# Gram products of two heads at once from a cleared buffer, in a one-core delta-rule attention and mixture kernel

## The reference, cut to what matters

```
B, H, S, D = 4, 8, 768, 48
k_n = k / (norm(k) + 1e-6)
for t in range(S):                       # state is [B, H, D, D], zero at first
    y[t]  = q[t] @ state
    state = state + beta[t] * outer(k_n[t], v[t] - k_n[t] @ state)
x = y as [3072, 384]
logits = x @ phi; d = softmax over tokens; c = softmax over the 32 slots
slots  = d.T @ x; slot_out = relu(slots @ w1[e]) @ w2[e];  x = c @ slot_out
h = x @ w_in; g = h * sigmoid(1.702 h); out = g @ w_out
```

## Time and profile before

| | |
|---|---|
| median of 3 runs | 500.15 us |
| profiled execution | 499.79 us, span 498.1 us |
| PE (matmul) busy | 462.5 us, 93% |
| PEld (weight load) busy | 344.1 us, 69% |
| VectorE (DVE) busy | 347.3 us, 70% |
| ScalarE (ACT) busy | 312.5 us, 63% |
| DMA moved | 59.20 MB, mean 119 GB/s |

### The profile page before, as it was taken

How to read it: one execution, slowest core, us unless ns; L and a number is a source line. 1 busy time by engine, 2 the same in 40 slices (tenths; PEclk the granted TensorE clock), 3 DMA queues, 4 the chain that set the end, 5 groups by cost and what they waited for, 6 DMA issues and landing times.

```text
span 498.1 us, 17806 instructions
## 1 busy us (share of the span) xinstructions
PE 462.5 (93%) x7422; PEld 344.1 (69%) x7422; DVE 347.3 (70%) x1126; ACT 312.5 (63%) x704; POOL 8.7 (2%) x21
## 2 busy tenths in 40 slices
PE   7889898978798899998999999999999999999997
PEld 4666675665566576665344788888788888887885
DVE  4985779999989998545652887566565656665662
ACT  3235657988869898875361776655656556556553
POOL 3000000000000000000000000000000000000000
PEclk8556888999989999999999999999999999999999
DMA  6911223666644434699999000100100100101001
GB/s 231 378 55 42 94 92 120 210 186 189 187 120 129 144 103 131 201 276 329 347 409 384 11 2 0 65 0 1 63 0 3 60 0 21 42 0 38 27 1 63
DMA packets 29800, 59.20 MB, mean 119 GB/s; under 512 B 3488, under 2 KB 12704, under 8 KB 29344
## 3 DMA queue, kind: packets, MB, share of 16 engines
q1 hardware_dynamic: 29728, 58.16, 34.4%
HBM read 53.43 MB, written 4.72 MB: 117 GB/s over the span
## 4 chain that ended last, share of the span: by engine, by line
PE 68%; DVE 17%; ACT 5%; issue 4%; DVEq 0%; ACTq 0%
PE bank L922 13%; PE bank L923 13%; PE bank L929 12%; DVE tmp L1273 5%; DVE tt L1278 5%; PE bank L889 4%; PE bank L612 3%; PE bank L552 3%; PE bank L625 2%; PE bank L819 2%; PE bank L794 2%; PE bank L541 2%; ACT zb L936 2%; ACT state L936 2%; DVE rr L1174 2%
## 5 line engine op out<-in xcount | busy, mean ns | idle before, releaser
L922 PE MATMUL bank<-g_h,wo_h 128*128 128x512 f32 x288 | 112.9, 392 | 0.1
L923 PE MATMUL bank<-g_h,wo_l 128*128 128x512 f32 x288 | 112.1, 389 | 0.0
L1497 DVE TENSOR_TENSOR g_l<-g,g_h 128x512 fp32r<-128x512 f32 x96 | 66.5, 693 | 64.6 <-ACT g_h L936 64.6
L936 ACT ACTIVATE g_h<-g 128x512 fp32r<-128x512 f32 x96 | 60.8, 634 | 69.2 <-DVE g L1492 69.2
L929 PE MATMUL bank<-g_l,wo_h 128*128 128x512 f32 x270 | 75.9, 389 | 0.0
L1492 DVE TENSOR_TENSOR g<-bank,sig 128x512 f32<-128x512 f32 x96 | 66.3, 691 | 13.1 <-ACT sig L1114 7.5
L936 ACT ACTIVATE zb<-bank 32x192 f32<-32x192 f32 x192 | 61.8, 322 | 17.2 <-PE bank L612 15.3
L1114 ACT ACTIVATE sig<-bank 128x512 f32<-128x512 f32 x96 | 57.2, 596 | 16.6 <-PE bank L889 16.2
L922 PEld LDWEIGHTS bank<-g_h,wo_h 128*128 128x128 f32 x288 | 54.1, 188 | 14.2 <-ACT res L936 2.6
L923 PEld LDWEIGHTS bank<-g_h,wo_l 128*128 128x128 f32 x288 | 54.1, 188 | 10.8
L1278 DVE TENSOR_TENSOR tt<-tt,tmp 128x126 f32<-128x126 f32 (+34 forms) x290 | 60.2, 250 | 0.0
(11 more groups left out here) (158 smaller groups left out, 485.7 us busy)
## 6 DMA issues: line engine op xcount, KB each, us to landing
slice<-in_w SPq DMA_DIRECT2D x48, 256.0 KB, 3.1
slice<-in_w SPq DMA_DIRECT2D x28, 384.0 KB, 7.0
kq<-in_kq_t SPq DMA_DIRECT2D x12, 512.0 KB, 6.6
kq<-in_kq_t SPq DMA_DIRECT2D x24, 256.0 KB, 3.1
vn<-in_v_nat SPq DMA_DIRECT2D x24, 192.0 KB, 3.1
out_t<-res SPq DMA_DIRECT2D x18, 256.0 KB, 2.1
kn<-in_k_nat SPq DMA_DIRECT2D x23, 192.0 KB, 2.7
win<-in_w_in SPq DMA_DIRECT2D x3, 1024.0 KB, 15.6
```

Source lines behind the costliest of these rows:

```text
L922: eng.matmul(acc[d][:], wo_h[:, f, cols], g_h[:, f % GR], start=(f == 0), stop=False)
L923: eng.matmul(acc[d][:], wo_l[:, f, cols], g_h[:, f % GR], start=False, stop=False)
L936: return eng.activation(out, src, ACT.Copy)
L1497: eng.tensor_tensor(g_l[:, f % GR], g[:, f % GR], g_h[:, f % GR].bitcast(F32), ALU.subtract).then_inc(s_gl, 1)
```

## The change

`kq` is split. k of 12 chunks and q of 4 chunks share a ring `kqa` of 16 places; a second buffer `sg` holds two chunks, [128, 2, 2 (a), 2 (k, q), 16 pairs, 32]. In its block a = 0 only partitions 0 to 63 are ever loaded and 64 to 127 stay zero (GpSimd clears them once); in block a = 1 the other way round. So one product with all 128 rows of k stationary and the 128 columns (two heads, k and q) of `sg` moving gives both heads' Gram products: 16 products of 128 columns in place of 32 of 64. This holds for chunks 4 to 23; chunks 0 to 3 keep the old form.

- Loads: per chunk one of k (256 KB), one of q (256 KB, now four chunks ahead, after `p_q`), and from chunk 4 on two more of 64 partitions each (256 KB each) for `sg`. In the start the `sg` loads of chunks 6 to 9 wait for the Grams of chunks 4 to 7.
- Filling products: the Grams of chunks 5 to 12 are each preceded by one product of 128 x 128 by 512 columns. `warm_up` has two products in place of one and is released at an earlier column.
- Order on TensorE: the Gram is one piece and stands after `update(c,0)`; `whole_block(c+1)` stands after `ks(c+1,0)`; in chunk 0 the Grams of chunks 9 and 10 stand after `pz(0)`.
- VectorE and ScalarE read out the Grams of chunks 8 and 9 later in chunk 0. GpSimd clears `sg` before `tt`.
- Expert weights: none in chunk 12, group (2, .) in chunks 13 to 16, (3, 0..2) in 17 to 19, (3, 3) at chunk 20.

```
-WARM_AT = 8 + 4 * 10
+QR, PR, QQ, QS = 12, 12, 4, 2
+WARM_AT = 8 + 4 * 5
+FILLED = CR + 1, 3 * CR + 1
...
+            def load_pair(c, a):
+                rows = slice(64 * a, 64 * a + 64)
+                eng.dma_start(sg[rows, c % QS, a], kq_t[c, rows]).then_inc(s_sg[c % QS], DMA)
...
             for c in range(CR, GA):
-                load_kq(c)
-            for c in range(3):
+                load_k(c)
+                if c >= CR + QS:
+                    eng.wait_ge(p_g, c - QS + 1)
+                for a in range(2):
+                    load_pair(c, a)
+                if c == CR + QS:
+                    load_vn(0)
+            load_kn(0)
+            for c in range(1, 3):
                 load_vn(c)
                 load_kn(c)
...
+                if c + QQ < NCH:
+                    eng.wait_ge(p_q, c + 1)
+                    load_q(c + QQ)
...
+                if c == 0:
+                    for n in range(GF, GA + 1):
+                        eng.wait_ge(p_g, n + 1)
+                        for a in range(2):
+                            load_pair(n + QS, a)
+                elif c + GA + QS < NCH:
+                    eng.wait_ge(p_g, c + GA + 1)
+                    load_pair(c + GA + QS, 0)
+                    eng.wait_ge(p_s, 2 * c + 2)
+                    load_pair(c + GA + QS, 1)
...
+            for a in range(2):
+                eng.memset(sg[64 - 64 * a:128 - 64 * a, :, a], 0.0).then_inc(z_sg, 1)
...
+                else:
+                    if FILLED[0] <= c < FILLED[1]:
+                        data = kqa[:, kslot(c)].rearrange("p b n -> p (b n)")
+                        eng.matmul(gp[gram_bank(c)].rearrange("p g n -> p (g n)"), data[:, 0:P], data, start=True, stop=True,
+                                   skip_group_check=True)
+                    for b in range(B):
+                        for q in range(HG):
+                            i = eng.matmul(gp[gram_bank(c)][quarter(q), 2 * b:2 * b + 2].rearrange("p a n -> p (a n)"),
+                                           kqa[:, kslot(c), pair_of(b, q)], sg[:, c % QS, :, :, pair_of(b, q)],
+                                           start=True, stop=True, skip_group_check=True)
+                i.then_inc(p_g, 1)
...
             eng.wait_ge(v_c, WARM_AT)
-            warm_up(1)
+            warm_up(2)
...
+                if c < LAST:
+                    update(c, 0)
                 if c == 0:
-                    for a in range(2):
-                        gram(GF, a)
-                    update(c, 0)
-                    for a in range(2):
-                        gram(GF + 1, a)
-                else:
-                    if ahead:
-                        gram(c + GA, 0)
-                    if c < LAST:
-                        update(c, 0)
-                    if ahead:
-                        gram(c + GA, 1)
-                if c + 1 < CR:
-                    whole_block(c + 1, ALL)
+                    gram(GF)
+                elif ahead:
+                    gram(c + GA)
...
                     ks(c + 1, 0)
+                    if c + 1 < CR:
+                        whole_block(c + 1, ALL)
...
                 if c == 0:
-                    for a in range(2):
-                        gram(GA, a)
+                    for n in range(GF + 1, GA + 1):
+                        gram(n)
```

More of the change, by code:

```diff
@@ L256, in program @@
         s_phi, s_beta = sems("s_phi s_beta")
-        s_kq = [sem(f"s_kq{i}") for i in range(QR)]
+        s_k = [sem(f"s_k{i}") for i in range(QR)]
+        s_q = [sem(f"s_q{i}") for i in range(QQ)]
+        s_sg = [sem(f"s_sg{i}") for i in range(QS)]
         s_kn = [sem(f"s_kn{i}") for i in range(3)]
@@ L433, in _ @@
                     load_expert_half(*expert, 0)
+                if c == 0:
[8 more added lines that the diff above has]
+                    load_pair(c + GA + QS, 1)
+                if c == NCH - CR:
+                    eng.wait_ge(p_k, 2 * c)
+                    for h in range(2):
+                        load_expert_half(3, EG - 1, h)
                 if NCH - CR <= c < LAST:
@@ L523, in warm_up @@
             def warm_up(n):
-                data = kq[:, ring(0)].rearrange("p a b n -> p (a b n)")
+                data = kqa[:, kslot(0)].rearrange("p b n -> p (b n)")
                 for _ in range(n):
[L526 to L535, removed]
-                else:
[L537 to L543, removed]
+                    eng.matmul(rz[1][:], data[:, 0:P], data, start=True, stop=True)
@@ new lines, in gram @@
+            def gram(c):
+                eng.wait_ge(s_k[c % QR], DMA * (c // QR + 1))
+                if c < CR:
+                    eng.wait_ge(s_q[c], DMA)
+                else:
+                    eng.wait_ge(s_sg[c % QS], 2 * DMA * ((c - CR) // QS + 1))
+                    eng.wait_ge(z_sg, 2)
+                if gram_before(c):
+                    eng.wait_ge(a_gk, gram_before(c))
+                    eng.wait_ge(v_p, gram_before(c))
+                if c < CR:
+                    for a in range(2):
+                        if a:
+                            eng.wait_ge(p_g0, c + 1)
+                        rows = slice(64 * a, 64 * a + 64)
+                        for b in range(B):
+                            for q in range(HG):
+                                i = eng.matmul(gp[gram_bank(c)][quarter(q), 2 * b + a], kqa[rows, kslot(c), pair_of(b, q)],
+                                               kqa[rows, qslot(c):kslot(c) + 1:QQ, pair_of(b, q)], start=True, stop=True,
+                                               skip_group_check=True)
+                        if a == 0:
+                            i.then_inc(p_g0, 1)
+                else:
+                    if FILLED[0] <= c < FILLED[1]:
+                        data = kqa[:, kslot(c)].rearrange("p b n -> p (b n)")
+                        eng.matmul(gp[gram_bank(c)].rearrange("p g n -> p (g n)"), data[:, 0:P], data, start=True, stop=True,
+                                   skip_group_check=True)
+                    for b in range(B):
+                        for q in range(HG):
+                            i = eng.matmul(gp[gram_bank(c)][quarter(q), 2 * b:2 * b + 2].rearrange("p a n -> p (a n)"),
+                                           kqa[:, kslot(c), pair_of(b, q)], sg[:, c % QS, :, :, pair_of(b, q)],
+                                           start=True, stop=True, skip_group_check=True)
+                i.then_inc(p_g, 1)
@@ L556, in qs @@
             def qs(c):
+                if c >= QQ:
+                    eng.wait_ge(s_q[c % QQ], DMA * (c // QQ + 1))
                 if c:
@@ L1360, in _ @@
                 columns = (*steps[0],) if r < NR else ()
-                for j in columns[:4] if c == 0 else columns[:2]:
+                for j in columns[:2]:
                     eliminate(r, j)
-                if c == 0:
-                    masked(GF)
                 if c and c - 1 + GA < NCH:
@@ L1368, in _ @@
                     turn_out(eng, eng.tensor_copy, turns[0])
-                for j in columns[4:] if c == 0 else columns[2:]:
+                for j in columns[2:]:
                     eliminate(r, j)
                 if c == 0:
-                    masked(GF + 1)
+                    masked(GF)
                 if c + 1 < CR:
```

62 lines of the change are left out of this document (36 added, 26 removed).

## The result

| | before | after |
|---|---|---|
| median of 4 runs each | 499.81 us | 514.78 us |
| lowest to highest | 496.77 to 500.9 | 511.35 to 517.5 |
| profiled execution (span) | 499.79 (498.1) | 513.41 (511.7) |

The ratio is 1.0306, with a 95% interval of 1.0224 to 1.0387. Forecast were 500.4 us and a range of 496.2 to 504.2; the result lies outside.

What follows compares the result with a forecast made beforehand. TensorE was taken to bound chunks 0 to 2, VectorE's elimination the stretch from chunk 3. Terms 1.6 - 1.2 + 0 + 0.8 - 0.8 + 0.1 = +0.5 on 499.79 gave 500.3, with run offset 500.4 us; range 496.2 to 504.2.

Steps and rivals of the forecast that it cites:

- What bounds: Whole kernel: the change can pay in the 40 us of chunks 0 to 2 and little elsewhere.
- forecast -0.8: Chunks 3 to 19: VectorE hides the Gram, but a gap and half clock in chunk 11 may shrink, -0.8 us.
- The Gram itself: Each new Gram on TensorE: 1.05 us at full clock against 1.43, 0.4 us less; a filling adds 0.85 to 1.04.
- The start, +1.6: Before chunk 0: `ks(0,0)` comes late because Gram 7 waits for its `sg` loads, 1.0 us per 64-partition load; +1.6 us.
- Rival B: Start: Gram 7 waits for `sg` loads that wait for Gram 5, 1.3 us per load; 502.9 us, chance 0.25.
- The rule of the ports: Start: partitions 0 to 63 reach half the ports, so a 64-partition load takes 1.2 us; sum 0.8 us higher.
- Chunk 0, -1.2: Chunk 0: 15.7 us against 17.38 at full clock, -1.7, less a possible clock fall; -1.2 us taken.
- A: Rival: clock stays at 2.4 GHz from Gram 5 through chunk 2, loads at full rate; 495.7 us, chance 0.27.
- Chunk 1, 0: Chunk 1: filling +0.45, fewer instructions and no half clock -0.95, later whole block +0.4; about 0.
- Chunk 2, +0.8 net: Chunk 2: update, ks and filling ahead of the moved block product cost +1.2; chunk 3 starts sooner, net +0.8 us.
- The loads in the loop, 0: Chunks 3 to 19: `sg` loads add 1.3 to 2.6 us of DMA per chunk, all with slack; 0 us.
- Chance: Whole kernel: odds of faster 0.33, same 0.35, slower 0.32, from the forecast and its rivals.

Runs made afterwards that it cites:

- e6: Changed kernel with `sg` loaded over all 128 partitions, no filling products, and the second block product at its old place; ratio 1.0101.
- e4: Kernel before with the six 512 KB start loads of chunks 4 to 9 each split in two loads of 64 partitions; ratio 1.0078.
- e9: Changed kernel with `sg` as a ring of four places in the same space, zero places left out; ratio 1.0300.
- e3: Changed kernel with the second block product of chunks 1 to 3 back at its old place, ahead of `update(c,1)`; ratio 1.0232.
- e1: Changed kernel with each `sg` load over all 128 partitions, half the bytes per partition, zero places not kept; ratio 1.0267.
- e8: Changed kernel without the `sg` loads of chunks 10 to 19, whose Grams read the chunk's own keys instead; ratio 1.0234.
- e15: Changed kernel without filling products and with the second block product at its old place, `sg` loads still of 64 partitions; ratio 1.0170.
- e10: Kernel before with added, unread loads of 64 partitions where the changed kernel loads `sg` of chunks 10 to 15; ratio 1.0048.

## Why the prediction was wrong, by its own steps

- **What bounds.** Right. The change could act in the start and in chunks 0 to 2 only, and did; chunks 3 to 11 took 71.5 us against 72.0, forecast -0.8.
- **The Gram itself.** Right in size: 1.05 and 1.9 us forecast, 1.08 and 1.94 measured; the filling 0.85 to 1.04 and 2.08 forecast, 1.10 to 1.13 and 2.04 measured. What was wrong was its worth: in e6 TensorE's matmuls take 31.4 us instead of 36.9, but the gaps rise from 3.1 to 6.5, and at most 1.4 us in 40 are left, no more than the profiles of the old code spread.
- **The start, +1.6: the step that failed most (+8.4).** The price of a 64-partition load, 1.0 us, was not far off by itself: 1.13 measured in e4. But chunk 4 was to be there at 14.2 (9.4 + 2.1 + 2.65) and landed at 17.97. Of these 3.8 us, 1.8 are the release: the third Gram, which lets the loads go, came at 11.23 instead of 9.40. The other 2.0 are the load: 6.74 us from issue to landing for k and two halves, forecast 4.75. The release was put at before's single 9.40 with nothing for the cut of the first four chunks' loads in two, which reach 289 GB/s from 2 to 8 us where before had 360. That cut explains about 0.8 of the 1.8, by the medians: the seven profiles without it have the release at 8.6 to 10.6 (median 10.3), the ten with it at 10.4 to 11.4 (median 11.1). From there the miss grows to Gram 7's end at 32.3 instead of 25.3: 0.8 in chunk 5's loads, 1.5 in the filled Gram 5 at half clock, 0.7 in chunk 7's loads, 0.2 in Gram 7. And the Gram's fillings were put at a rising clock; two of three ran at 2.04 and 2.08 us. Rival B had the mechanism and the bound (1.3 us), and still gave 502.9, since it used the same release time. Its wait for the Gram of chunk 5 is what the trace shows ahead of Gram 7, but to take it away gains nothing, since the queue alone gives the same landing (e9).
- **The rule of the ports** (the Trainium skill, SBUF — State Buffer, "Door 1: The DMA port swizzle": half of the partitions reach half of the ports), weighed in the prediction against rows that showed only full loads, holds here: 231 and 234 GB/s by halves against 404 and 395, and two halves in the queue together move no more. By the 1.2 us estimated from the page's figure the sum would have been 0.8 higher, which is a small part of the miss.
- **Chunk 0, -1.2 (+1.8).** Here the clock was to pay for the fillings. It was at 0.50 again from 38 to 48 us, and three fillings took 4.2 us. A fell with it. The estimate also kept two gaps at 1.3 us together; one alone is 1.76.
- **Chunk 1, 0 (+1.2).** The gap of 1.79 us at 62.92, and 3.64 us in which VectorE waits for the moved block product (0.73 before; but 3.98 in e3, where it is at its old place).
- **Chunk 2, +0.8 net (+2.35).** Mechanism right, size too small: the wait is 5.47, forecast about 3.5 (2.27 + 1.2). Missing are the gap of 1.18 and the half clock of the filled Gram; in e1 and e8, without these two, the moved block leaves chunk 2 at 11.6.
- **The loads in the loop, 0.** This is the second step that failed: "all have a chunk of slack". So they have in the changed kernel, for those who read them (in e15 one Gram stands 1.10 us for its load). But beside them TensorE's waits for its next piece of program grow, from 3.1 to 4.8 us in chunks 0 to 2. How much of that is the loads' doing in the changed kernel stays open; in the kernel before the same loads raise them to 4.3 and cost 2.4 us in all (e10).
- **Chance.** Slower had 0.32 and nothing above 506.7. The terms were bounded one by one; that the start's terms stand in series, and that all went the same way once the queue was full, was not.

## What to carry to other kernels

A load that is cut in two costs by what it releases: count it up to the first step that its end allows, and take the release time from more than one profile. Cost every load that is added, the ones "with slack" too: data that nobody waited for cost this kernel 0.48%. Where a gap is called "issue", look for what landed just before it ended, a load or a piece of program. A product that fills TensorE to raise its clock has to be shorter than what the higher clock gives back before the next thin stretch: here six fillings of 1.1 to 2.1 us, up to the end of chunk 0, bought back 0.8 us for each of two or three Grams. On an engine in written order, price a moved step with all that now stands ahead of it at its worst length, not at its usual one.

## What the runs showed of the hardware that was not expected

- Loads of 64 partitions move 231 and 234 GB/s with the DMA engines as full (1.03 and 1.04, e4) as at 404 and 395; two of them on the two halves, issued one behind the other, are no faster together.
- TensorE stands after some 250 or 500 matmul records until 1.2 to 1.6 us after a 16 KB packet of its program has landed (48 of 49 gaps in chunks 0 to 2). The gaps are 0.4 to 3.8 us long; in all they were 2.6 and 3.1 us there in before, and 4.2 and 4.3 with loads added that nobody reads.
- A PEclk of 1.00 can mean that the trace has no clock record for that time: the changed kernel's begins at 27.6 us, and ahead of it stand fillings of 2.04 us (1.10 at 2.4 GHz). The lengths decide.
- Two profiles of the same kernel differ by 1.4 us in the start and 0.5 us in a chunk: a single profile does not carry a difference under 1 us.
